# The last normalising turns of an attention stage moved behind the first matmuls of the next stage

## The chip, the core and the metric

The kernel runs on one core of a Trainium2 chip. The metric is the device time of one execution in microseconds (us). Engines of the core work side by side, each through its own queue in program order: TensorE (PE; its weight loads are shown apart as PEld), VectorE (DVE), ScalarE (ACT), GpSimd (POOL) and SyncE, which issues most DMAs (SPq). They wait for each other by semaphores.

## The reference

Three stages follow each other. Cut to what matters:

```
def _attn_ref(q, k, v, w1, b1, w2):          # 4 batches, 8 heads, 576 positions, 64 wide
    scores = scale * q @ k.T
    x = log1p(|i - j|) / log1p(max(i, 1))
    scores += (relu(x @ w1 + b1) @ w2)        # a bias for each head
    attn = exp(scores - max); attn /= sum(attn) + 1e-9
    return attn @ v
def _moe_ref(x, w_in, w_out):                 # 2304 tokens, 512 -> 2048 -> 512
    h = x @ w_in
    return (h - tanh(h)) @ w_out
def _moe2_ref(x, w_gate, w1, w2):             # one of 8 experts for each token
    e = argmax(x @ w_gate); g = softmax(x @ w_gate)[e]
    return g * (relu(x @ w1[e]) @ w2[e])
```

## The kernel before, in words

The three stages run in order: bias and attention, the dense layer with the routing, and the experts. The change lies in the attention stage and at its seam with the dense layer.

Attention works on 16 pairs of heads (`PAIRS_A`, pair `g`), each in 5 tiles of queries (`QT`; `rows(t)` is 128 for the first four and 64 for the last). For each step PE forms the scores of the next tile, turns the probabilities of this one by transposes into the PSUM banks `pt_a`, `pt_b` and `misc`, and multiplies those of an earlier pair with v into `o_acc` (`values_main`, `values_rest`). The output is kept transposed, so that queries lie along the free axis. The inverse row sums therefore have to be turned too: VectorE computes them (`inverse`, L665 and L667), repeats each over 64 columns (`widen`, L676, tile `at_inv_wide`), and PE transposes that tile by tile (`turn_inverse`, L464). VectorE multiplies the output copied from PSUM (`copy_main` L693, `copy_rest` L699, tile `at_o_sb`) with the turned inverses (`scaled`, L687) into `at_x_sb`, which SyncE stores to `x_dram`. The last pair has the number `LASTP`, 15. In the loop the turns of pair g come some steps later, one in each step; those of the last tile come once for each pair. After the loop the turns and products of the last two pairs stand written out.

The dense layer works on chunks of 384 tokens (`CH` is 3 tiles) and, within a chunk, on 16 slots m of 128 hidden columns. `up(m)` (L1009) is 12 matmuls of 384 columns into one of three banks, `down(m)` (L1054) is 9 matmuls of 512 columns. All operands are split in a high and a low half: `split_x_high` (ScalarE, L958) and `split_x_low` (VectorE, L963) for the tokens, `split_second_low` (L995) for a piece of the weights. Between `up` and `down` of a slot ScalarE squares (L1169, L1171), and takes the tanh and a mask (L1175, L1179); VectorE runs four operations (L1261, L1268, L1272, L1274), ScalarE takes the high half (L1185) and VectorE the low half (L1257). The seam is overlapped by hand: the attention function itself calls `dense.first_up`, which is `up(0)` and `up(1)`, at the end of its PE program, and the splits of the first chunk at the end of those of ScalarE and VectorE. The dense layer then issues `up(m+2)` ahead of `down(m)`. VectorE's first dense operation stands in its queue behind the two last `scaled` of pair 15.

SyncE at the seam, in its order: the store of pair 14, a piece of weights (`load_third_weights`), the second chunk of x, the store of pair 15 after the wait for its products (L385), a wait for all stores (L387), nine small loads and stores, and the next piece of weights (L935).

Of the kernel before, what the change touches and what calls it, by code (L numbers as in the profile page):

```python
# [26 lines left out]
P = 128  # L27
# [18 lines left out]
def rows(t):  # L46

    return P if t < QT - 1 else LAST
# [105 lines left out]
def bias_and_attention(nc, stay, mem, w1, b1, w2, dist, psi, rpsi_rows, bias_dram, q, k, v, ident, x_dram):  # L154
# [10 lines left out]
    with ExitStack() as ctx:  # L165
        def sem(name):
            return stay.enter_context(nc.semaphore("at_" + name))

        def buf(name, shape, dt=F32):
            return ctx.enter_context(nc.sbuf_tensor("at_" + name, shape, dt))  # L170
# [34 lines left out]
        id_sb, id_in = mem.id_sb, mem.id_in  # L205
# [4 lines left out]
        inv_wide = [buf(f"inv_wide{i}", [P, QT, 2 * D]) for i in range(2)]  # L210
# [24 lines left out]
        turn_done = sem("turn_done")  # L235
# [51 lines left out]
        def turn_of(g, t):  # L287

            p, tile = (g - 1, 0) if t == QT - 1 else (g - 2, t + 1)
            return (p, tile) if real(p) and g < PAIRS_A else None  # L290
# [98 lines left out]
        def tensor(pe, dense):  # L389
# [40 lines left out]
            def values(g, slot, o, at, queries):  # L430

                j_a, j_b = (slot, MID + 1 + slot) if slot < MID else (MID, MID)
                for c, j in ((0, j_a), (1, j_b)):
                    keys = slice(0, P) if j != MID else slice(c * D, (c + 1) * D)
                    last = nc.tensor.matmul(o[c * D:(c + 1) * D, at:at + queries.stop - queries.start],  # L435
                                            v_nat[g % NV][keys, j, :], prob_t[g % 2][keys, j, queries],
                                            start=slot == 0, stop=slot == MID)
                return last

            def values_main(g, slot):  # L440
                if slot == 0:
                    pe.wait_ge(v_in[g % NV], 16 * (g // NV + 1))
                    pe.wait_ge(pta_read, QT * g + QT - 1)
                    pe.wait_ge(ptb_read, QT * g + QT - 1)
                    pe.wait_ge(mid_read, QT * g + QT - 1)
                    if g:
                        pe.wait_ge(o_read, g)
                last = values(g, slot, o_acc, 0, slice(0, MAIN))
                if slot == MID:
                    last.then_inc(o_done, 1)  # L450

            def values_rest(g, bank, at):
                pe.wait_ge(pta_read, QT * (g + 1))
                pe.wait_ge(ptb_read, QT * (g + 1))
                pe.wait_ge(mid_read, QT * (g + 1))
                for slot in range(MID + 1):
                    last = values(g, slot, bank, at, slice(MAIN, S))
                last.then_inc(rem_done, 1)

            def turn_inverse(p, tile, bank, at):  # L460

                if tile == 0:
                    pe.wait_ge(widened, p + 1)
                nc.tensor.transpose(bank[:, at:at + P], inv_wide[p % 2][:, tile, :], id_sb[:, :]).then_inc(turn_done, 1)  # L464

            def misc_free(g, t):

# [19 lines left out]
            for g, t in STEPS:  # L487
                n = g * QT + t
                if real(g) and real((n + 1) // QT):
                    scores((n + 1) // QT, (n + 1) % QT)  # L490
                if not real(g):
                    continue
                pe.wait_ge(prob_done[0], n + 1)
                if n:
                    pe.wait_ge(pta_read, n)
                for j in range(MID):
                    last = turn_prob(pt_a, j * P, n, j)
                last.then_inc(pta_done, 1)
                if t == QT - 1:
                    values_main(g, 0)  # L500
                elif real(g - 1):
                    values_main(g - 1, t + 1)
                pe.wait_ge(prob_done[1], n + 1)
                if n:
                    pe.wait_ge(ptb_read, n)
                for j in range(MID + 1, KTP):
                    last = turn_prob(pt_b, (j - MID - 1) * P, n, j)
                last.then_inc(ptb_done, 1)
                misc_free(g, t)
                if turn_of(g, t):  # L510
                    turn_inverse(*turn_of(g, t), misc, TURN_AT)
                if t == QT - 1 and real(g - 1):
                    values_rest(g - 1, misc, REM)
                turn_prob(misc, 0, n, MID).then_inc(mid_done, 1)
# [3 lines left out]
            for tile in range(1, QT - 1):  # L518
                turn_inverse(LASTP - 1, tile, misc, tile * P)
            pe.wait_ge(pta_read, QT * PAIRS_A)  # L520
            turn_inverse(LASTP - 1, QT - 1, pt_a, 0)
            for slot in range(1, MID + 1):
                values_main(LASTP, slot)
            values_rest(LASTP, pt_b, 0)
            pe.wait_ge(x_done, QT * LASTP)
            for tile in range(QT - 1):
                turn_inverse(LASTP, tile, misc, tile * P)
            turn_inverse(LASTP, QT - 1, pt_a, 0)
            dense.first_up(pe)

        def scalar(act, dense):
            act.dma_start(dist_sb[:, :], dist).then_inc(dist_in, 16)
# [92 lines left out]
        def vector(dve, dense):  # L625
# [36 lines left out]
            def inverse(p):  # L662
                dve.wait_ge(prob_done[0], QT * (p + 1))
                dve.wait_ge(prob_done[1], QT * (p + 1))
                nc.vector.tensor_scalar_add(guarded[:, :, :], total[p % 2][:, :, :], 1e-9).then_inc(norm_step, 1)  # L665
                dve.wait_ge(norm_step, 2 * p + 1)
                nc.vector.reciprocal(inv[p % 2][:, :, :], guarded[:, :, :]).then_inc(norm_step, 1)  # L667

            def widen(p):

                dve.wait_ge(norm_step, 2 * p + 2)
                if p >= 2:
                    dve.wait_ge(turn_done, QT * (p - 1))
                one = inv[p % 2][:, :, :]
                many = bass.AP(one.tensor, one.offset, [one.ap[0], [1, 2 * QT], [0, D]])
                nc.vector.tensor_copy(inv_wide[p % 2][:, :, :].rearrange("p t (c d) -> p (t c) d", d=D), many).then_inc(widened, 1)  # L676

            def scaled(p, tile, tiles, bank, at):
                m = (tiles - 1) * P + rows(tile + tiles - 1)
                cols = slice(tile * P, tile * P + m)  # L680
                if tile <= 1 and p >= 2:
                    dve.wait_ge(x_out[p % 2], 16 * (p // 2))
                dve.wait_ge(turn_done, QT * p + tile + tiles)
                dve.wait_ge(o_read, p + 1)
                if tile + tiles == QT:
                    dve.wait_ge(rem_read, p + 1)
                nc.vector.tensor_tensor(x_sb[p % 2][:, cols], o_sb[:, cols], bank[:, at:at + m], ALU.mult).then_inc(x_done, tiles)  # L687

            def copy_main(p):
                if p:  # L690
                    dve.wait_ge(x_done, QT * p - 1)
                dve.wait_ge(o_done, p + 1)
                nc.vector.tensor_copy(o_sb[:, 0:MAIN], o_acc[:, :]).then_inc(o_read, 1)  # L693

            def copy_rest(p, bank, at):
                if p:
                    dve.wait_ge(x_done, QT * p)
                dve.wait_ge(rem_done, p + 1)
                nc.vector.tensor_copy(o_sb[:, MAIN:S], bank[:, at:at + LAST]).then_inc(rem_read, 1)  # L699
# [22 lines left out]
            for g, t in STEPS:  # L722
                n = g * QT + t
                m = rows(t)
# [22 lines left out]
                if turn_of(g, t):  # L747
                    p, tile = turn_of(g, t)
                    scaled(p, tile, 1, misc, TURN_AT)
                if t == QT - 1 and real(g - 1):  # L750
                    copy_rest(g - 1, misc, REM)
            for j in range(CH):
                dense.split_x_low(dve, 0, j)
            scaled(LASTP - 1, 1, QT - 2, misc, P)
            scaled(LASTP - 1, QT - 1, 1, pt_a, 0)
            inverse(LASTP)
            widen(LASTP)
            dense.split_second_low(dve)
            copy_main(LASTP)
            copy_rest(LASTP, pt_b, 0)  # L760
            scaled(LASTP, 0, QT - 1, misc, 0)
            scaled(LASTP, QT - 1, 1, pt_a, 0)

        return Attention(sync, tensor, scalar, vector, over, banks_read, turned)


# [4 lines left out]
CH = 3  # L771
# [1336 lines left out]
```

## Time and profile before

| what | us |
|---|---|
| device time, three runs | 1053.72, 1054.59, 1055.21 |
| median | 1054.59 |
| the profiled execution: device time | 1053.72 |
| its span, first to last instruction | 1051.8 |
| PE busy in the span | 1012.9 (96%) |
| VectorE, ScalarE busy | 689.2 (66%), 631.2 (60%) |

The 1.9 us between the span and the device time lie outside the first and last instruction. The attention stage reaches to about 346 us, the dense layer begins there. A busy PE means that a matmul is in its pipeline; in a stream of matmuls the distance of starts tells the pace, and the duration of one is longer than that distance.

### The profile page before, as it was taken

The numbers are of one execution on the slowest core, as the hardware profiler recorded it, in microseconds if no ns is written. First come the engines' busy times: TensorE is split into PE (matmuls) and PEld (weight loads), VectorE is DVE, ScalarE is ACT, GpSimd is POOL, SyncE is SP. The second block draws the span as 40 slices with busy tenths as digits, with TensorE's granted clock in tenths as the row PEclk, the third lists the DMA queues.
The fourth block names the chain that finished last, engine by engine and source line by source line (L and its number), as shares of the span: only waits on it lengthen the run. The fifth ranks groups of instructions, "written<-read, shape, count | busy, mean of one in ns | idle before, by whom it ended". The sixth has DMA issues, their size and how long they took to land. (4 is left out here: it accounts for less than half of the span.)

```text
span 1051.8 us, 19004 instructions
## 1 busy us (share of the span) xinstructions
PE 1012.9 (96%) x6540; PEld 787.9 (75%) x6540; DVE 689.2 (66%) x1570; ACT 631.2 (60%) x1340; POOL 87.3 (8%) x134
## 2 busy tenths in 40 slices
PE   6889999999999999999999999999998999999995
PEld 2256666666665789988988989888877888888884
DVE  7987878787888896766757657668754442632321
ACT  6987777777777685666566556567732432732421
POOL 0000000000000000000100100001023231331221
PEclk9999999999999999999999999999999999999998
DMA  7771252422512530010100100201115351631111
GB/s 227 265 250 56 71 168 71 160 81 65 148 46 94 183 111 1 31 31 31 31 1 31 31 1 31 81 31 58 40 51 205 122 195 40 215 102 40 36 40 36
DMA packets 62094, 92.15 MB, mean 88 GB/s; under 512 B 24486, under 2 KB 29990, under 8 KB 61990
## 3 DMA queue, kind: packets, MB, share of 16 engines
q1 hardware_dynamic: 56806, 79.32, 22.9%
q0 software_dynamic: 4192, 11.07, 3.3%
q8 instruction: 52, 0.85, 0.3%
q10 hardware_dynamic: 1008, 0.61, 0.2%
q14 instruction: 36, 0.29, 0.1%
HBM read 66.19 MB, written 25.73 MB: 87 GB/s over the span
## 5 line engine op out<-in xcount | busy, mean ns | idle before, releaser
L1009 PE MATMUL score<-dl_xt,dl_weights 128*128 128x384 f32 x1152 | 219.8, 339 | 0.0
L1009 PEld LDWEIGHTS score<-dl_xt,dl_weights 128*128 128x128 f32 x1152 | 202.1, 188 | 8.5 <-issue 3.0
L574 ACT ACTIVATE at_prob<-at_neg,at_negmax 128x576 f32<-128x576 f32 (+1 forms) x160 | 123.6, 773 | 54.2 <-DVE at_negmax L657 40.2
L1169 ACT ACTIVATE dl_val<-score 128x384 f32<-128x384 f32 x96 | 47.1, 490 | 131.3 <-PE score L1009 125.9
L1261 DVE SCALAR_TENSOR_TENSOR dl_sq<-dl_sq,dl_val 128x384 f32<-128x384 f32 x96 | 53.5, 557 | 99.3 <-ACT dl_sq L1171 97.7
L657 DVE CUSTOM_DVE_ANT_0 at_neg<-score,at_bias 128x576 f32<-128x576 f32 (+1 forms) x160 | 114.2, 750 | 2.2 <-PE score L420 1.7
L1814 PE MATMUL o_acc<-dl_weights,ex_ht_hi 128*128 128x512 f32 x336 | 109.1, 405 | 0.9 <-ACT ex_y_sb L1899 0.9
L1784 PE MATMUL score<-dl_weights,ex_xt_hi 128*128 128x512 f32 x336 | 105.6, 395 | 0.0
L435 PE MATMUL o_acc<-at_prob_t,at_v_nat 128*64 128x512 f32 (+1 forms) x320 | 85.7, 616 | 1.2 <-DVE at_o_sb L693 1.2
L428 PEld LDWEIGHTS pt_b<-id_sb,at_prob 128*128 128x128 f32 (+1 forms) x320 | 32.0, 140 | 63.5 <-ACT at_prob L574 48.1
L1479 POOL DMA_INDIRECT slot_dram<-slot_rows,slot_i x18 | 17.8, 987 | 727.5 <-DVE slot_i L1342 723.9
L1784 PEld LDWEIGHTS score<-dl_weights,ex_xt_hi 128*128 128x128 f32 x336 | 61.5, 188 | 12.2 <-issue 0.2
L1814 PEld LDWEIGHTS o_acc<-dl_weights,ex_ht_hi 128*128 128x128 f32 x336 | 60.0, 188 | 12.5 <-ACT ex_y_sb L1899 1.1
L1814 PE MATMUL o_acc<-dl_weights,ex_ht_lo 128*128 128x512 f32 x168 | 66.2, 394 | 0.0
L1784 PE MATMUL score<-dl_weights,ex_xt_lo 128*128 128x512 f32 x168 | 65.7, 391 | 0.0
L1054 PE MATMUL o_acc<-dl_weights,dl_g_hi 128*128 128x512 f32 x192 | 60.6, 396 | 1.9 <-DVE dl_g_lo L1257 1.6
L1171 ACT ACTIVATE dl_sq<-dl_val,minus_b 128x384 f32<-128x384 f32 x96 | 59.3, 618 | 3.1
L420 PE MATMUL score<-at_k_hi,at_q_hi 64*128 64x288 f32 x320 | 58.0, 340 | 2.6 <-DVE at_negmax L657 2.0
L1272 DVE COPY_PREDICATED dl_sq<-dl_over,dl_big 128x384 f32<-128x384 uint32 x96 | 57.8, 602 | 3.5 <-DVE dl_sq L1268 0.2
L1054 PE MATMUL score<-dl_weights,dl_g_hi 128*128 128x512 f32 x192 | 59.8, 392 | 0.0
L1054 PE MATMUL pt_b<-dl_weights,dl_g_hi 128*128 128x512 f32 x192 | 59.3, 390 | 0.0
L1179 ACT ACTIVATE dl_over<-dl_val,minus_small 128x384 f32<-128x384 f32 x96 | 58.2, 606 | 0.0
(222 smaller groups left out, 1985.8 us busy)
## 6 DMA issues: line engine op xcount, KB each, us to landing
dl_raw<-in_moe_w SPq DMA_DIRECT2D x12, 1024.0 KB, 7.6
ex_raw_b<-in_moe_w SPq DMA_DIRECT2D x8, 1024.0 KB
at_bias<-bias_dram SPq DMA_DIRECT2D x3, 2304.0 KB, 10.2
bias_dram<-at_prob SPq DMA_DIRECT2D x20, 288.0 KB, 2.1
at_k_all<-in_k SPq DMA_DIRECT2D x16, 288.0 KB, 3.5
at_q_all<-in_q SPq DMA_DIRECT2D x16, 288.0 KB, 4.2
at_v_nat<-in_v SPq DMA_DIRECT2D x16, 288.0 KB, 3.1
bias_dram<-at_rows_sb SPq DMA_DIRECT2D x16, 288.0 KB, 3.6
```

The lines of the kernel that those rows point to most:

```text
L420: last = nc.tensor.matmul(score[c][:, half, 0:HALF], a[g % 2][part, cols], b[g % 2][part, keys], start=i == 0, stop=i == 2)
L435: last = nc.tensor.matmul(o[c * D:(c + 1) * D, at:at + queries.stop - queries.start], v_nat[g % NV][keys, j, :], prob_t[g % 2][keys, j, qu ...
L574: nc.scalar.activation(prob[n % 2][0:m, c, :], neg[c][n % 2][0:m, :], ACT.Exp, bias=negmax[c][n % 2][0:m, 0:1], scale=-1.0, accum_out=tota ...
L657: nc.vector.tensor_tensor_reduce(out=neg[c][n % 2][0:m, :].rearrange("p (a c) -> p a c", a=2), in0=score[c][0:m, :, 0:HALF], in1=bias[hp % ...
L1009: last = nc.tensor.matmul(h_ps[m % NHB][:, 0:CN], w[f // KT][:, k, fc], x[c % 2][:, k, :], start=k == 0 and n == 0, stop=k == KT - 1 and n ...
L1054: last = nc.tensor.matmul(x2_ps[j][:, :], g[m % 2][:, tok], w[f // KT][:, f % KT, :], start=f == 0 and n == 0, stop=f == FT - 1 and n == 2)
L1171: nc.scalar.activation(sq[m % 2][:, :], val[m % 2][:, :], ACT.Square, bias=minus_b[:, 0:1], scale=SQ_A).then_inc(sq_done, 1)
L1179: nc.scalar.activation(over[m % 2][:, :], val[m % 2][:, :], ACT.Relu, bias=minus_small[:, 0:1]).then_inc(over_done, 1)
L1261: nc.vector.scalar_tensor_tensor(out=sq[m % 2][:, :], in0=sq[m % 2][:, :], scalar=SQ_C, in1=val[m % 2][:, :], op0=ALU.add, op1=ALU.mult).t ...
L1272: nc.vector.copy_predicated(s[:, :], over[m % 2][:, :].bitcast(mybir.dt.uint32), big[m % 2][:, :]).then_inc(dve_step, 1)
L1784: last = nc.tensor.matmul(h_ps[half][:, :], x[:, k, :], w1_of(r, half, w)[:, k, :], start=k == 0 and n == 0, stop=k == KT - 1 and n == 2)
L1814: last = nc.tensor.matmul(y_ps[:, :], x[:, half * KT + k, :], weights[:, r % 2, half, w, k, :], start=half == 0 and k == 0 and n == 0, sto ...
```

## The change

Three edits, all in `bias_and_attention`. `turn_inverse` transposes only the rows of the tile, so 64 by 64 of the identity for the last tile of a pair. `dense.first_up` stands before the turns of the last pair on PE. On VectorE the three `split_x_low` of the first chunk stand behind `widen(LASTP)`.

```
-                nc.tensor.transpose(bank[:, at:at + P], inv_wide[p % 2][:, tile, :], id_sb[:, :]).then_inc(turn_done, 1)
+                m = rows(tile)
+                nc.tensor.transpose(bank[:, at:at + m], inv_wide[p % 2][0:m, tile, :], id_sb[0:m, 0:m]).then_inc(turn_done, 1)
...
             values_rest(LASTP, pt_b, 0)
+            dense.first_up(pe)
             pe.wait_ge(x_done, QT * LASTP)
             for tile in range(QT - 1):
                 turn_inverse(LASTP, tile, misc, tile * P)
             turn_inverse(LASTP, QT - 1, pt_a, 0)
-            dense.first_up(pe)
...
-            for j in range(CH):
-                dense.split_x_low(dve, 0, j)
             scaled(LASTP - 1, 1, QT - 2, misc, P)
             scaled(LASTP - 1, QT - 1, 1, pt_a, 0)
             inverse(LASTP)
             widen(LASTP)
+            for j in range(CH):
+                dense.split_x_low(dve, 0, j)
             dense.split_second_low(dve)
```

PE's queue at the seam, before: the turns of pair 14, its last products with v, the turns of pair 15, then three `up`.

```order
L464 MATMUL misc<-id_sb,at_inv_wide 128x128 x3
L464 MATMUL pt_a<-id_sb,at_inv_wide 128x128
L435 MATMUL o_acc<-at_prob_t,at_v_nat 64x512 x8
L435 MATMUL pt_b<-at_prob_t,at_v_nat 64x64 x10
L464 MATMUL misc<-id_sb,at_inv_wide 128x128 x4
L464 MATMUL pt_a<-id_sb,at_inv_wide 128x128
L1009 MATMUL score<-dl_xt,dl_weights 128x384 x36
L1054 MATMUL o_acc<-dl_weights,dl_g_hi 128x512 x2
```

The same place now (line numbers behind the edit are one higher):

```order
L465 MATMUL misc<-id_sb,at_inv_wide 128x128 x3
L465 MATMUL pt_a<-id_sb,at_inv_wide 128x64
L435 MATMUL o_acc<-at_prob_t,at_v_nat 64x512 x8
L435 MATMUL pt_b<-at_prob_t,at_v_nat 64x64 x10
L1010 MATMUL score<-dl_xt,dl_weights 128x384 x24
L465 MATMUL misc<-id_sb,at_inv_wide 128x128 x4
L465 MATMUL pt_a<-id_sb,at_inv_wide 128x64
L1010 MATMUL score<-dl_xt,dl_weights 128x384 x12
```

Two of the three `up` (24 matmuls) stand ahead of the five turns of pair 15; the third stays behind them.

VectorE's queue at the seam, before. `dl_xt` is the low half of the tokens, `dl_sq` the first dense operation of slot 0.

```order
L699 COPY at_o_sb<-misc 128x64
L963 TENSOR_TENSOR dl_xt<-dl_x_nat,dl_xt 128x4x128 x3
L687 TENSOR_TENSOR at_x_sb<-at_o_sb,misc 128x384
L687 TENSOR_TENSOR at_x_sb<-at_o_sb,pt_a 128x64
L665 TENSOR_SCALAR at_guarded<-at_total 128x10
L667 RECIPROCAL at_inv<-at_guarded 128x10
L676 COPY at_inv_wide<-at_inv 128x640
L995 TENSOR_TENSOR dl_weights<-dl_raw,dl_weights 128x2048
L693 COPY at_o_sb<-o_acc 128x512
L699 COPY at_o_sb<-pt_b 128x64
L687 TENSOR_TENSOR at_x_sb<-at_o_sb,misc 128x512
L687 TENSOR_TENSOR at_x_sb<-at_o_sb,pt_a 128x64
```

The same place now, as far as the first dense operation of slot 0:

```order
L700 COPY at_o_sb<-misc 128x64
L688 TENSOR_TENSOR at_x_sb<-at_o_sb,misc 128x384
L688 TENSOR_TENSOR at_x_sb<-at_o_sb,pt_a 128x64
L666 TENSOR_SCALAR at_guarded<-at_total 128x10
L668 RECIPROCAL at_inv<-at_guarded 128x10
L677 COPY at_inv_wide<-at_inv 128x640
L964 TENSOR_TENSOR dl_xt<-dl_x_nat,dl_xt 128x4x128 x3
L996 TENSOR_TENSOR dl_weights<-dl_raw,dl_weights 128x2048
L694 COPY at_o_sb<-o_acc 128x512
L700 COPY at_o_sb<-pt_b 128x64
L688 TENSOR_TENSOR at_x_sb<-at_o_sb,misc 128x512
L1262 SCALAR_TENSOR_TENSOR dl_sq<-dl_sq,dl_val 128x384
```

The three `split_x_low` stand behind five attention operations. The two products of pair 15 keep their place ahead of the first dense operation.

## Rows read from the trace of the kernel before

**Rows 1.** The page: busy time, share of the span, instructions.
```profile
PE 1012.9 (96%) x6540; PEld 787.9 (75%) x6540; DVE 689.2 (66%) x1570; ACT 631.2 (60%) x1340; POOL 87.3 (8%) x134
```

**Rows 2.** Waits of PE after 350 us: total us, times, longest.
```profile
PE score L1797 <- DVE ex_h_sb L1965: 1.8, 1, 1.8
PE o_acc L1054 <- DVE dl_g_lo L1257: 1.6, 2, 0.9
PE misc L1773 <- DMA ex_x_sb<-x_dram,dl_tile_rows: 1.6, 2, 1.3
PE o_acc L1814 <- ACT ex_y_sb L1899: 0.9, 1, 0.9
```

**Rows 3.** Timeline of PE at the seam: start, duration, instructions, idle before.
```profile
340.44 0.52 PE L464 MATMUL misc<-id_sb,at_inv_wide 128*128 128x128 f32 x3 [0.97 <-DVE at_o_sb L699]
...
345.60 0.66 PE L464 MATMUL misc<-id_sb,at_inv_wide 128*128 128x128 f32 x4
346.09 0.27 PE L464 MATMUL pt_a<-id_sb,at_inv_wide 128*128 128x128 f32 x1
346.12 6.49 PE L1009 MATMUL score<-dl_xt,dl_weights 128*128 128x384 f32 x36
353.50 0.70 PE L1054 MATMUL o_acc<-dl_weights,dl_g_hi 128*128 128x512 f32 x2 [0.89 <-DVE dl_g_lo L1257]
```

**Rows 4.** Timeline of DVE at the seam.
```profile
339.96 0.22 DVE L699 COPY at_o_sb<-misc 128x64 f32<-128x64 f32 x1
340.27 1.90 DVE L963 TENSOR_TENSOR dl_xt<-dl_x_nat,dl_xt 128x512 fp32r<-128x512 f32 x3
342.09 0.55 DVE L687 TENSOR_TENSOR at_x_sb<-at_o_sb,misc 128x384 f32<-128x384 f32 x1
...
343.55 2.28 DVE L995 TENSOR_TENSOR dl_weights<-dl_raw,dl_weights 128x2048 fp32r<-128x2048 f32 x1
...
346.56 0.69 DVE L687 TENSOR_TENSOR at_x_sb<-at_o_sb,misc 128x512 f32<-128x512 f32 x1
347.17 0.21 DVE L687 TENSOR_TENSOR at_x_sb<-at_o_sb,pt_a 128x64 f32<-128x64 f32 x1
349.72 0.56 DVE L1261 SCALAR_TENSOR_TENSOR dl_sq<-dl_sq,dl_val 128x384 f32<-128x384 f32 x1 [2.34 <-ACT dl_sq L1171]
```

**Rows 5.** Timeline of ACT, first dense slot and two weights pieces.
```profile
348.55 0.49 ACT L1169 ACTIVATE dl_val<-score 128x384 f32<-128x384 f32 x1 [5.45 <-PE score L1009]
349.07 0.62 ACT L1171 ACTIVATE dl_sq<-dl_val,minus_b 128x384 f32<-128x384 f32 x1
...
356.27 1.91 ACT L1198 ACTIVATE dl_weights<-dl_raw 128x2048 fp32r<-128x2048 f32 x1
...
365.18 1.91 ACT L1200 ACTIVATE dl_weights<-dl_raw 128x2048 fp32r<-128x2048 f32 x1
```

**Rows 6.** Timeline of PE in the loop: turns of 128 and of 64.
```profile
282.13 0.27 PE L464 MATMUL misc<-id_sb,at_inv_wide 128*128 128x128 f32 x1
282.24 0.27 PE L428 MATMUL misc<-id_sb,at_prob 128*128 128x128 f32 x1
...
283.42 0.40 PE L428 MATMUL pt_a<-id_sb,at_prob 64*128 64x64 f32 x4
283.75 1.08 PE L435 MATMUL o_acc<-at_prob_t,at_v_nat 128*64 128x512 f32 x4
```

**Rows 7.** Groups of PEld by shape, 92 to 340 us: count, busy, mean ns.
```profile
L464 PEld LDWEIGHTS misc<-id_sb,at_inv_wide 128*128 128x128 f32 x71 | 9.9, 140 | 1.0
L428 PEld LDWEIGHTS pt_a<-id_sb,at_prob 64*128 64x128 f32 x56 | 5.5, 137 | 0.2 <-issue 0.2
```

**Rows 8.** SyncE's queue at the seam.
```profile
347.41 0.33 SPq L385 DMA_DIRECT2D x_dram<-at_x_sb  x1
352.21 0.37 SPq L1023 DMA_DIRECT2D dl_gate_sb<-in_moe_w_gate  x1
356.34 0.59 SPq L935 DMA_DIRECT2D dl_raw<-in_moe_w_in  x1
```

**Rows 9.** DMA issues 343 to 357 us: KB each, us to landing.
```profile
dl_raw<-in_moe_w_in SPq DMA_DIRECT2D x1, 1024.0 KB, 5.5
```

**Rows 10.** Windows: length, busy of PE, PEld, DVE, ACT, POOL, granted clock, DMA.
```profile
0.00:10.00 10.00, 1.51 (x10) 0.90 (x14) 4.87 (x20) 3.81 (x7) 0.21 (x5) 1.00 0.78 223
200.00:300.00 100.00, 99.77 (x842) 62.15 (x840) 79.74 (x242) 73.96 (x211) 0.00 (x0) 1.00 0.38 117
1045.00:1052.00 7.00, 0.00 (x0) 0.00 (x0) 0.00 (x0) 0.00 (x0) 0.00 (x0) 0.59 0.04 13
```

**Rows 11.** Timeline of PE, first idle time of the program.
```profile
9.07 5.81 PE L401 MATMUL score<-at_feat,at_w_blk 128*32 128x288 f32 x64 [2.19 <-DMA at_w_blk<-in_w]
```

More of the change, by code:

```diff
@@ L463, in turn_inverse @@
                     pe.wait_ge(widened, p + 1)
-                nc.tensor.transpose(bank[:, at:at + P], inv_wide[p % 2][:, tile, :], id_sb[:, :]).then_inc(turn_done, 1)
+                m = rows(tile)
+                nc.tensor.transpose(bank[:, at:at + m], inv_wide[p % 2][0:m, tile, :], id_sb[0:m, 0:m]).then_inc(turn_done, 1)
             def misc_free(g, t):
@@ L524, in tensor @@
             values_rest(LASTP, pt_b, 0)
+            dense.first_up(pe)
             pe.wait_ge(x_done, QT * LASTP)
@@ L528, in tensor @@
             turn_inverse(LASTP, QT - 1, pt_a, 0)
-            dense.first_up(pe)
         def scalar(act, dense):
@@ L751, in vector @@
                     copy_rest(g - 1, misc, REM)
-            for j in range(CH):
-                dense.split_x_low(dve, 0, j)
             scaled(LASTP - 1, 1, QT - 2, misc, P)
@@ L757, in vector @@
             widen(LASTP)
+            for j in range(CH):
+                dense.split_x_low(dve, 0, j)
             dense.split_second_low(dve)
```

## The prediction

> **What bounds the kernel now.** I read the page first: PE is busy 96% of the span [rows 1], and in the attention loop 99.77 of 100 us [rows 10]. So the time is PE's stream, and a change counts by what it takes out of that stream or by the holes it opens or closes in it. The waits of PE behind 350 us come next: a few us in all, and the one the change touches is `down(0)`, which waits for the low half of slot 0 from VectorE, 0.89 us at 353.50 [rows 2, 3]. The rest of the dense layer has almost no hole. The reader should then lay the timelines of the seam side by side. On PE the five turns of pair 15 start at 345.60 and `up(0)` at 346.12, 0.52 us later; three `up` run 6.49 us, to 352.61; PE then waits until 353.50 [rows 3]. On ScalarE the square of slot 0 starts at 348.55, after `up(0)` [rows 5]. On VectorE the last products of pair 15 end at 347.38, it sits idle 2.34 us, and the chain of slot 0 starts at 349.72 [rows 4]. The start of that chain sets `down(0)`: 353.50 - 349.72 = 3.78 us lie between them. What moves 349.72 moves everything behind it, since PE has no spare time there to catch up.
>
> **Part 1: `first_up` ahead of the turns.** `up(0)` starts where the turns did, 345.60, a gain of 0.52 us for the tokens' side: ScalarE's square would start at 348.03 and its second square would end at 349.69 - 0.52 = 349.17 [rows 5]. If VectorE were free, its chain would start 0.5 us earlier than before. It is not. The queue of VectorE is in program order, and ahead of its first dense operation stand the two products of pair 15, which need the turns. These now come after 24 matmuls. The pace of `up` is (6.49 - about 0.35 for the last one) / 35 = 0.175 us, so 24 take 4.2 us and the turns start at 345.60 + 4.2 = 349.8. The four into `misc` last 0.66 us [rows 3], to 350.45. With 0.05 us for the signal VectorE starts the large product at 350.5; the next one starts 0.61 us later (347.17 - 346.56), and the operation behind that about 0.13 us later (0.21 us long, overlapping its successor, as the small ones do) [rows 4]. The chain of slot 0 then starts at 350.5 + 0.61 + 0.13 = 351.24 in place of 349.72: 1.5 us late. `down(0)` comes at 351.24 + 3.78 = 355.0. PE has the same five turns and three `up` to do, ready at 352.6, so the hole of 0.89 us grows to 2.4 us. This term is +1.5 us, bounded by -0.5 (VectorE not held at all) and +1.8 (a signal of 0.2 us and a full 0.21 for the small product). I take +1.5.
>
> **Part 2: `split_x_low` later.** VectorE is free of the 128x64 copy at 340.18, but the product of pair 14 needs turns that PE starts at 340.44 and ends at 340.96 [rows 3, 4]. So it waits some 0.8 us, starts at 341.0 in place of 342.09, and the five small operations, which took 343.55 - 342.09 = 1.46 us, end at 342.5. The three splits (1.9 us) end at 344.4 in place of 342.17. `up(0)` needs them at 345.60: 1.2 us of cover. The split of the weights, 2.28 us, ends at 346.7, and the two copies behind it, which took from 345.83 to 346.56, at 347.5 [rows 4], under the wait for the turns at 350.5. SyncE gets pair 14 a microsecond earlier and the second load of x at about the same time as before. All of it is hidden; cost 0. If the cover were gone, each 0.1 us beyond 1.2 would delay `up(0)`, yet even then the order of events behind it is set by the turns, and they would shift with it.
>
> **Part 3: smaller turns.** Each of 16 pairs has one last tile; 14 of its turns lie in the loop, two at the end. Two 128-wide turns in the loop start 0.11 us apart, and four 64 by 64 turns of the same form take 0.33 us to the next group, 0.083 each [rows 6]. The difference is 0.03 us, and since PE is the bound there, it is time: 16 x 0.03 = 0.48, of which the one of pair 15 now lies ahead of the hole and gives nothing. I take -0.4. The ends are 0 (the load of weights binds) and 16 x 0.055 = -0.9 (the turn costs half).
> The loads of 64 rows last 137 ns where those of 128 last 140 [rows 7]. The Trainium skill, page "TensorE: Matmul & The Clock Gate", section "LDWEIGHTS (loading the stationary operand)", says that a load goes by its columns and not its rows, which these two rows bear out. It gives 107 ns for 128 columns; if that bound the turns, this term would be nothing and the sum +1.5. The 0.083 us of the 64 by 64 turns, which load 128 columns each, speaks against it as the binding limit.
>
> **Part 4: the store of pair 15.** It was issued at 347.41 and is now issued when its products end, at about 351.5. SyncE waited from there to 352.21 for it, 4.4 us and more, then took 4.13 us for nine small transfers and issued the next weights at 356.34 [rows 8], which landed 5.5 us later [rows 9], at 361.8. ScalarE needs them at 365.18 [rows 5], 366.7 when shifted. By the same waits again the weights would come at 351.5 + 4.8 + 4.1 + 5.5 = 365.9, still 0.8 us early, and probably earlier, since the large loads that the store queued behind are through by 351.5. Cost 0. ScalarE's own wait for all stores stands ahead of the weights at 356.27 [rows 5], about 357.8 now, and the store is in by 356.3 at worst.
>
> **Sum.** +1.5 - 0.4 = +1.1 us. Against the profiled execution, 1053.72, that is 1054.8. That execution was the fastest of three, 0.87 below the median, and the difference carries over to the median: 1054.59 + 1.1 = 1055.7.
>
> **Rivals.**
> - *The small turns save nothing*, by the weight load or because PE's instruction issue binds there. For it: the loads of weights last as long for 64 rows as for 128 [rows 7]. Against it: the 0.083 above. +1.5, so 1056.1.
> - *Given back later*: some later hole is set by something that doesn't move, a DMA or POOL, and takes up the 1.5 us. The holes of rows 2 name `ex_x_sb` from a gather, 1.6 us in all; but that gather waits for work that shifts with PE. Then only -0.4 is left: 1054.2.
> - *VectorE isn't held*, because the turns come through sooner than the queue suggests. The 0.5 us are gained and 0.4 on top: 1053.7. Against it: PE starts matmuls in the queue's order all along the timeline.
> - *Slower side, the clock falls in the wider hole.* The idle 2.19 us at the start passed at a granted clock of 1.00, level 2.4 GHz [rows 10, 11], and only the 7 idle us at the end show 0.59, so partly 1.2 GHz [rows 10]. The hole here would be 2.4 us with PE busy before it. It decides only if the wider hole makes the clock fall, which no row here tells. If one slot (`up` and `down`, 4.25 us from 353.50 to 357.75 in the loop's pace) ran at half the clock, it would add 4.2 us: 1059.9. The Trainium skill, same page, section "HAM oscillation — how this bites in real kernels", warns that idle gaps between bursts bring the slower level back.
> - *SyncE's queue is late*: the weights of part 4 miss the 0.8 us of cover by up to 1 us: 1056.7.
>
> **Chances.** The forecast 0.60, with 1054.8 to 1056.7 as its own range; small turns for nothing 0.15; given back 0.08; not held 0.05; clock 0.07; SyncE late 0.05. About 0.2% (2.1 us) is what a measurement of this kernel can tell from no change, so slower means above 1056.7 and faster below 1052.5. Slower: all of the clock's 0.07, 0.03 of SyncE's, 0.08 from the upper tails of the first two, 0.18. Faster: 0.04, tails of the third and fourth. The same: 0.78. The range, 1054.0 to 1057.3, leaves the clock and the outer tails out.
>
> **What would show it.** In the profile after: `up(0)` directly behind the last products with v at about 345.2 (0.4 less for the small turns); the turns of pair 15 between the second and third `up`; VectorE idle for about 3 us ahead of the product 128x512 with PE's turn named as what it waited for, and the chain of slot 0 right behind the small product with no wait for ScalarE; a hole of about 2.4 us before `down(0)`; the rest of the dense layer as before, shifted by 1.1 us. A hole under 1 us would refute the first term, `up(0)` starting still at 345.6 the third; PE's clock under 1.00 around 355 us would make the clock rival true.

## The result and the profile after

The changed kernel takes 1059.91 us (median of 5, 1058.96 to 1062.35) where the kernel before took 1054.59 (1053.72 to 1055.21). The ratio is 1.0053, 95% interval 1.0043 to 1.0064: slower by 5.3 us. The forecast was 1055.7, with a range of 1054.0 to 1057.3. The profiled execution took 1059.48 us, its span is 1057.6, 5.8 us over the span of before.

The timeline of PE at the seam shows where [rows 3]; columns as there. The third row is the last turn in the loop; before, it stood at 339.19.

```profile
338.46 0.27 PE L465 MATMUL misc<-id_sb,at_inv_wide 64*128 64x64 f32 x1
338.66 0.33 PE L428 MATMUL misc<-id_sb,at_prob 128*128 128x128 f32 x1
...
342.30 0.27 PE L428 MATMUL misc<-id_sb,at_prob 64*128 64x64 f32 x1
343.54 0.52 PE L465 MATMUL misc<-id_sb,at_inv_wide 128*128 128x128 f32 x3 [0.97 <-DVE at_o_sb L700]
...
348.80 4.44 PE L1010 MATMUL score<-dl_xt,dl_weights 128*128 128x384 f32 x24
353.07 0.60 PE L465 MATMUL misc<-id_sb,at_inv_wide 128*128 128x128 f32 x4
353.60 0.27 PE L465 MATMUL pt_a<-id_sb,at_inv_wide 64*128 64x64 f32 x1
353.81 2.35 PE L1010 MATMUL score<-dl_xt,dl_weights 128*128 128x384 f32 x12
358.37 0.70 PE L1055 MATMUL o_acc<-dl_weights,dl_g_hi 128*128 128x512 f32 x2 [2.21 <-DVE dl_g_lo L1258]
...
361.25 3.10 PE L1010 MATMUL score<-dl_xt,dl_weights 128*128 128x384 f32 x12
364.19 0.63 PE L1055 MATMUL o_acc<-dl_weights,dl_g_hi 128*128 128x512 f32 x2
```

The first turn of inverses in the loop, in the changed kernel and in the kernel before, and further rows of before:

```profile
93.67 0.33 PE L465 MATMUL misc<-id_sb,at_inv_wide 128*128 128x128 f32 x1
```
```profile
92.58 0.33 PE L464 MATMUL misc<-id_sb,at_inv_wide 128*128 128x128 f32 x1
...
339.19 0.27 PE L428 MATMUL misc<-id_sb,at_prob 64*128 64x64 f32 x1
...
355.64 2.27 PE L1009 MATMUL score<-dl_xt,dl_weights 128*128 128x384 f32 x12
357.75 0.63 PE L1054 MATMUL o_acc<-dl_weights,dl_g_hi 128*128 128x512 f32 x2
```

Read against the rows of before, four distances changed. The first turn of inverses in the loop starts at 93.67 and not 92.58: 1.1 us from the start of the program, which differs between executions. The kernel before and the one with the late splits alone, whose code is the same up to this turn, have it at 92.58 and 93.44. From that turn to the loop's last turn it is 248.63 us (93.67 to 342.30) where it was 246.61 (92.58 to 339.19): +2.0. From there to the first `down` it is 16.07 where it was 14.31: +1.8, with the hole grown from 0.89 to 2.21. And from the first `down` to the second it is 5.82 (358.37 to 364.19) where it was 4.25 (353.50 to 357.75): +1.6. The rows inside tell why: 12 matmuls of `up` last 3.10 us in place of 2.27. The windows give the granted clock there (the third value from the end, ahead of the DMA's two):

```profile
359.00:360.00 1.00, 1.00 (x6) 0.77 (x5) 0.97 (x3) 0.60 (x2) 0.00 (x0) 0.84 0.12 13
360.00:361.00 1.00, 1.00 (x4) 0.81 (x3) 0.88 (x3) 1.00 (x3) 0.00 (x0) 0.50 0.03 2
361.00:362.00 1.00, 1.00 (x5) 0.90 (x4) 0.97 (x2) 1.00 (x2) 0.00 (x0) 0.50 0.52 152
362.00:363.00 1.00, 1.00 (x5) 1.00 (x4) 0.60 (x2) 1.00 (x2) 0.00 (x0) 0.50 0.51 80
363.00:364.00 1.00, 1.00 (x7) 1.00 (x6) 0.83 (x1) 0.56 (x2) 0.00 (x0) 0.95 0.98 377
```

The clock fell to its lower level, 1.2 GHz, some 1.3 us after the hole's end (358.37; the window from 359 holds 0.84), and stayed there for some 3.4 us (0.16 + 3 x 0.50 + 0.05 = 1.7 us of lost clock). Behind the second `down` the rest of the program is 0.6 us shorter than before, no more than single executions differ.

VectorE's timeline answers to rows 4:

```profile
343.07 0.22 DVE L700 COPY at_o_sb<-misc 128x64 f32<-128x64 f32 x1
344.26 0.55 DVE L688 TENSOR_TENSOR at_x_sb<-at_o_sb,misc 128x384 f32<-128x384 f32 x1 [0.98 <-PE pt_a L465]
...
345.73 1.89 DVE L964 TENSOR_TENSOR dl_xt<-dl_x_nat,dl_xt 128x512 fp32r<-128x512 f32 x3
347.53 2.29 DVE L996 TENSOR_TENSOR dl_weights<-dl_raw,dl_weights 128x2048 fp32r<-128x2048 f32 x1
...
353.88 0.69 DVE L688 TENSOR_TENSOR at_x_sb<-at_o_sb,misc 128x512 f32<-128x512 f32 x1 [3.33 <-PE pt_a L465]
354.48 0.21 DVE L688 TENSOR_TENSOR at_x_sb<-at_o_sb,pt_a 128x64 f32<-128x64 f32 x1
354.62 0.55 DVE L1262 SCALAR_TENSOR_TENSOR dl_sq<-dl_sq,dl_val 128x384 f32<-128x384 f32 x1
```

It is held 3.33 us by PE's turn, and the chain of slot 0 starts right behind the two products, with no wait for ScalarE. The splits end at 347.62, 1.2 us ahead of `up(0)`.

### The profile page after: what moved, and what is told of

Same layout as the page of the kernel before. It is cut to its first block and busy times, and to the rows that moved or that the text cites. A ratio compares the mean times of both kernels' runs of the same rounds, so it can differ in the third digit from the quotient of the medians.

```text
span 1057.6 us, 19004 instructions
## 1 busy us (share of the span) xinstructions
PE 1018.5 (96%) x6540; PEld 790.7 (75%) x6540; DVE 689.2 (65%) x1570; ACT 631.5 (60%) x1340; POOL 88.8 (8%) x134
```

## The experiments

Times against the kernel before are differences of medians, with before run on the same chip beside them (1054.86, 1054.67 and 1054.86 us in the three series). "Loop" is the distance from the first turn of inverses to the last turn of the middle block, 246.61 us before; "seam" is from there to the first `down`, 14.31 us before.

**The small turns alone.** Only the first edit.

```
-                nc.tensor.transpose(bank[:, at:at + P], inv_wide[p % 2][:, tile, :], id_sb[:, :]).then_inc(turn_done, 1)
+                m = rows(tile)
+                nc.tensor.transpose(bank[:, at:at + m], inv_wide[p % 2][0:m, tile, :], id_sb[0:m, 0:m]).then_inc(turn_done, 1)
```

> The kernel before with only the 64 by 64 turns. Theory (the change of tile shape costs about 0.09 us on each side of a small turn): PE loses 0.14 to 0.15 us for each of 14 pairs in the loop, so +2.0 us against before, and the hole before the first down stays at 0.9 us with the clock at 1.00. Rival (the drift up to the seam in the changed kernel is the start of the execution, the small turns save what was forecast): 0 to -0.5 us.

Measured: 1057.06 us, +2.2, ratio 1.0018 (1.0009 to 1.0027). Loop 248.59 us (92.93 to 341.52), +2.0; the hole 0.89 us, the clock 1.00. The rival is out: less work on PE made the loop longer, by 0.14 us for each of the 14 small turns in it. The seam is 0.4 us longer as well, where two more small turns stand.

**The small turn at another place.** In the loop it stands behind the turn of the middle block, so that the scores, which use 64 rows, follow it. The semaphores that the two turns signal are exchanged with them.

```
...
-                if turn_of(g, t):
+                late = turn_of(g, t) and t == QT - 2
+                if turn_of(g, t) and not late:
                     turn_inverse(*turn_of(g, t), misc, TURN_AT)
...
-                turn_prob(misc, 0, n, MID).then_inc(mid_done, 1)
+                turn_prob(misc, 0, n, MID).then_inc(turn_done if late else mid_done, 1)
+                if late:
+                    turn_inverse(*turn_of(g, t), misc, TURN_AT, mid_done)
```

> The kernel before with 64 by 64 turns, where in the loop the small turn stands behind the turn of the middle block in place of ahead of it, so that its other neighbour is the scores, which work on 64 rows too. The two signals are exchanged with it. Theory (a change between 128 and 64 rows costs 0.09 us, and here the one to the scores is there anyway): within 0.7 us of before, the distance from the turn of the middle block to the scores longer by 0.05 us or less. Rival (a small turn is slow by itself, wherever it stands): +2.2 us as with the small turns alone.

Measured: 1055.28 us, +0.6, ratio 1.0005 (0.9996 to 1.0014). Loop 246.58 us (92.96 to 339.54): the 2.0 us are gone, with the same 64 by 64 turns. The seam is 16.39 us in the trace, 2.1 longer: 1.7 of it is a fall of the clock, shown in the last section, and 0.4 are the two small turns behind the loop, which stayed between wide ones.

Small turns aren't slow; their neighbours make them so. The starts of PE and of its weight loads (PEld) around one small turn show it. The changed kernel, with 128-row turns on both sides:

```profile
284.40 0.66 PE L428 MATMUL pt_b<-id_sb,at_prob 128*128 128x128 f32 x4
284.99 0.27 PE L465 MATMUL misc<-id_sb,at_inv_wide 64*128 64x64 f32 x1
285.19 0.33 PE L428 MATMUL misc<-id_sb,at_prob 128*128 128x128 f32 x1
285.45 0.40 PE L420 MATMUL score<-at_k_hi,at_q_hi 64*128 64x288 f32 x2
```
```profile
284.99 0.13 PEld L465 LDWEIGHTS misc<-id_sb,at_inv_wide 64*128 64x128 f32 x1 [0.17 <-issue]
285.19 0.14 PEld L428 LDWEIGHTS misc<-id_sb,at_prob 128*128 128x128 f32 x1
285.45 0.19 PEld L420 LDWEIGHTS score<-at_k_hi,at_q_hi 64*128 64x128 f32 x2
```

The kernel before at its counterpart of this place, PE and then PEld, where all the turns have 128 rows (the two turns behind this group are in [rows 6]):

```profile
281.64 0.66 PE L428 MATMUL pt_b<-id_sb,at_prob 128*128 128x128 f32 x4
...
282.55 0.40 PE L420 MATMUL score<-at_k_hi,at_q_hi 64*128 64x288 f32 x2
```
```profile
282.02 0.14 PEld L464 LDWEIGHTS misc<-id_sb,at_inv_wide 128*128 128x128 f32 x1
282.13 0.14 PEld L428 LDWEIGHTS misc<-id_sb,at_prob 128*128 128x128 f32 x1
```

Before, the load of a turn started at 282.02 and its matmul at 282.13: 0.11 us ahead, under the matmul in front. Between turns of different row counts the load starts together with its own matmul (284.99 and 284.99, 285.19 and 285.19), and the starts are 0.20 us apart in place of 0.11. The kernel before has such a step too, where scores of 64 rows follow a turn of 128: the turn starts at 289.54, the load and the first matmul of the scores both at 289.74. From the start of the group into `pt_b` to the scores it is 1.05 us where it was 0.91 (281.64 to 282.55); with the small turn behind the middle block it is 0.91 again (281.98 to 282.89). The Trainium skill ("TensorE: Matmul & The Clock Gate", "Part 3: Packing small matmuls — row/col tiling", The mechanism) states that a load overlaps with matmuls in flight "only when row_grp differs" (the group of rows that an instruction works on). In these traces the "only" doesn't hold: loads for equal 128-row tiles overlapped, and those between a 64-row and a 128-row tile, which share rows, didn't. The measurement decides.

**The two moves alone**, turns of 128 (second and third hunk of the change).

> The kernel before with only the two moves (first_up ahead of the turns of pair 15, the low splits behind widen), turns of 128. Theory (VectorE is held 1.5 us, and the clock falls in the wider hole): hole about 2.2 us, first down 1.3 to 1.8 us later, then about 3.4 us at a granted clock of 0.50, which costs 1.6 us more: +3.0 to +3.4. Rival (the clock's fall is not the hole's doing, or is no cost): +1.5. Rival (all of the loss is the order's): +5.3.

Measured: 1057.17 us, +2.3, ratio 1.0023 (1.0014 to 1.0032). Loop 246.64 us, seam 16.00, hole 2.47 us. The profiled execution kept its clock at 1.00. But the 11 executions form two groups: five from 1055.94 to 1056.33 us with a mean clock of 0.996 or 0.997, and six from 1057.17 to 1060.42 with 0.995 or 0.994. None of the three expectations is met as written. The lower group is +1.2 (median 1056.09), which is put down to the hole, and the upper one 1.5 more (median 1057.55), put down to a fall of the clock. That the upper six had a fall is inferred: only one execution of each kernel has a trace. The mean clock is a rough sign of it. The seven traces of this case without a fall before the end of the program show 0.996 or 0.997, the four with one show 0.996, so 0.996 can be either, and 0.995 is lower than any trace. Of the kernel before, run beside this one, 3 of 27 executions have 0.995 or less, of this kernel 6 of 11, of the changed kernel 16 of 30 (all its executions on record; the time above is the median of five).

**The late splits alone.** Only the third hunk.

> The kernel before with only the three low splits behind widen. Theory (they stay under the last products with v): 0, within 0.3 us, the first down as before and the hole 0.9 us. Rival (they delay the first up or the copies behind them and with them the chain of slot 0): +0.4 to +1.0 us, which would be part of what is put down to the moved turns.

Measured: 1054.70 us, -0.2, ratio 1.0000 (0.9991 to 1.0009); seam 14.31, hole 0.89. The splits are covered, and the 1.2 us belong to the moved turns.

**The turns between the first two `up`**, 128 wide, splits late. `first_up` takes the number of the `up` here.

```
+            dense.first_up(pe, 0)
             pe.wait_ge(x_done, QT * LASTP)
             for tile in range(QT - 1):
                 turn_inverse(LASTP, tile, misc, tile * P)
             turn_inverse(LASTP, QT - 1, pt_a, 0)
-            dense.first_up(pe)
+            dense.first_up(pe, 1)
```

> The kernel before with the low splits behind widen and the five turns of pair 15 (128 wide) between up(0) and up(1). Theory (the loss of the order is VectorE held by the products of pair 15 until the turns are through): up(0) starts 0.5 us earlier than before, the products run from about 0.8 us after the end of up(0), the chain of slot 0 starts 0.4 to 0.5 us earlier relative to the last products with v, the hole before the first down is 0.3 to 0.5 us, the clock stays at 1.00: -0.3 to -0.5 us, a difference that can hardly be told. Rival (the late splits or the moved up cost something of their own): +0.5 to +1.5.

Measured: 1053.96 us, -0.7, ratio 0.9996 (0.9987 to 1.0005): not to be told from before. In the trace the seam is 13.91 us, 0.4 shorter. VectorE now waits 1.15 us and not 3.33:

```profile
348.65 0.69 DVE L688 TENSOR_TENSOR at_x_sb<-at_o_sb,misc 128x512 f32<-128x512 f32 x1 [1.15 <-PE pt_a L464]
349.26 0.21 DVE L688 TENSOR_TENSOR at_x_sb<-at_o_sb,pt_a 128x64 f32<-128x64 f32 x1
349.39 0.55 DVE L1261 SCALAR_TENSOR_TENSOR dl_sq<-dl_sq,dl_val 128x384 f32<-128x384 f32 x1
```
```profile
353.16 0.70 PE L1054 MATMUL o_acc<-dl_weights,dl_g_hi 128*128 128x512 f32 x2 [0.41 <-DVE dl_g_lo L1257]
```

One `up` more or less ahead of the turns is the difference between a gain of 0.4 us at the seam and a loss of 1.7.

The clock did fall in this profiled execution, though not at the seam but in the expert stage, behind an idle time of 1.76 us. The rows of this kernel, its window, and the rows of before, where the same idle time passed at 1.00:

```profile
796.50 0.66 PE L1797 MATMUL score<-id_sb,ex_h_sb 128*128 128x128 f32 x4 [1.76 <-DVE ex_h_sb L1965]
...
804.66 0.66 PE L1773 MATMUL misc<-id_sb,ex_x_sb 128*128 128x128 f32 x4 [0.22 <-DMA ex_x_sb<-x_dram,dl_tile_rows]
```
```profile
798.00:801.00 3.00, 3.00 (x9) 2.33 (x8) 0.52 (x1) 0.00 (x0) 1.04 (x1) 0.50 1.00 369
```
```profile
796.93 0.66 PE L1797 MATMUL score<-id_sb,ex_h_sb 128*128 128x128 f32 x4 [1.76 <-DVE ex_h_sb L1965]
...
804.53 0.66 PE L1773 MATMUL misc<-id_sb,ex_x_sb 128*128 128x128 f32 x4 [1.27 <-DMA ex_x_sb<-x_dram,dl_tile_rows]
```

From the first of these rows to the last it is 8.16 us where it was 7.60, so this fall cost 0.6 us: PE's next wait, for a gather, shrank from 1.27 to 0.22 and gave the rest back.

**A hole in the kernel before.** Its own order, and VectorE kept busy by 5 more copies ahead of `copy_main(LASTP)`.

```
+            dve.wait_ge(o_done, PAIRS_A)
+            dve.wait_ge(x_done, QT * LASTP)
+            for n in range(5):
+                nc.vector.tensor_copy(o_sb[:, 0:MAIN], o_acc[:, :]).then_inc(held, 1)
+                dve.wait_ge(held, n + 1)
             copy_main(LASTP)
```

> The kernel before in its own order, with 5 copies of 128x512 added on VectorE ahead of copy_main(LASTP), some 3.3 to 3.6 us, of which 2.3 are covered. Theory: the hole before the first down grows to about 2.0 to 2.3 us with no other change, and the clock falls as in the changed kernel: +1.1 to +1.4 for the hole and +1.6 for the clock, together +2.8. Rival (it takes the moved turns to bring the clock down): clock 1.00 and +1.2.

Measured: 1056.98 us, +2.1, ratio 1.0016 (1.0007 to 1.0025). Seam 15.50, hole 2.05 us, clock 1.00 in the profiled execution, and again two groups: five executions from 1055.45 to 1056.15 with 0.996 or 0.997, and six from 1056.98 to 1058.74, four of these with 0.995, the others with 0.996 and 0.998. The first group is +0.6, its median 1055.46. So a hole of this size gives the same picture without the moved turns, less clearly: four of the six later executions have a mean clock lower than any trace, and the one with 0.998 must be late for another reason.

**The hole filled**, in the changed kernel and in the one with the two moves alone.

```
                     attention.banks_read(pe)
+                    for n in range(9):
+                        nc.tensor.matmul(x2_ps[0][:, :], win_hi[0][:, n % KT, 0:P], win_hi[0][:, n % KT, :], start=True, stop=True)
```

> The changed kernel with 9 matmuls of 512 columns put in the hole before the first down (about 2.0 us of PE work whose result is overwritten), nothing else. Theory (PE's idle time makes the clock fall): the granted clock stays at 1.00 behind 355 us and the time is 1.5 us under the changed kernel, so +3.7 against before. Rival (the clock falls for another reason, as the small turns or the phase of the execution): clock 0.50 for 3.4 us again and +5.3. Rival (the filling itself delays down): above +5.3.

Measured: 1058.63 us, +3.8, ratio 1.0035 (1.0022 to 1.0049); four of the five executions lie between 1058.45 and 1058.71, and none has a mean clock under 0.996. PE's row shows the filling and no idle time ahead of `down`, and the window behind it the clock at 1.00:

```profile
355.80 2.25 PE L1099 MATMUL o_acc<-dl_weights 128*128 128x512 f32 x9
357.98 0.73 PE L1055 MATMUL o_acc<-dl_weights,dl_g_hi 128*128 128x512 f32 x2
```
```profile
356.00:364.00 8.00, 8.00 (x38) 6.66 (x37) 7.06 (x13) 6.73 (x12) 0.00 (x0) 1.00 0.36 99
```

Nine matmuls whose result is thrown away make the changed kernel 1.3 us faster (1059.91 to 1058.63). None of its own 30 executions is under 1058.86.

> The two moves with turns of 128, as in the order-only kernel, and 10 matmuls of 512 columns in the hole before the first down (about 2.2 us of work whose result is overwritten). Theory (the fall of the clock comes from PE's idle time there, and comes only in part of the executions): the upper group of the order-only kernel (1057.2 and above, mean clock 0.994 to 0.995) is gone, all executions lie near its lower group, +1.2 to +1.5 us. Rival (the two groups come from something else): the same two groups again, 1.3 us apart.

Measured, with ten: 1056.42 us, +1.6, ratio 1.0015 (1.0006 to 1.0024). Nine of the 11 executions lie between 1055.63 and 1056.71; one of the 11 has a mean clock under 0.996, where it was six. Two are slower, 1057.48 and 1058.90, with 0.996. The first of these is the profiled one: its clock is 1.00 from 340 to 1040 us, and PE waits 3.1 us for the gather `ex_x_sb` where it was 1.6 [rows 2]. So the low-clock executions became rare with the hole filled, and single executions can be late for another reason.

**Both mended**, small turns behind the middle block and the last turns between the `up`.

> The two of this series together: small turns behind the turn of the middle block in the loop, and the turns of pair 15 between up(0) and up(1). Theory: the sum of the two, -1.0 to +0.2 us against before, no fall of the clock before the end. Rival (small turns slow by themselves): +1.7.

Measured: 1054.22 us, -0.5, ratio 0.9997 (0.9988 to 1.0006). Loop 246.62 us (92.69 to 339.31), seam 14.27, hole 0.41. Its profiled execution has a fall of the clock near 798 us as well, behind an idle time of 1.77 us. This and the turns between alone are the best of the series; neither beats the kernel before by more than the measurement can tell.

## Why the prediction was wrong

- **Part 1, `first_up` ahead of the turns: right.** Forecast +1.5 us with a hole of 2.4; measured 2.21 us of hole in the changed kernel, a seam longer by 1.7 us with the two moves alone, and +1.2 (their lower group) to +1.6 (hole filled) in the time. The mechanism is the one told: VectorE's queue holds the chain of slot 0 behind two products that wait for PE. Moving one `up` to the other side of the turns takes it away.
- **Part 2, late splits: right.** 0, and 1.2 us of cover as worked out.
- **Part 3, smaller turns: this step failed.** It stood at -0.4 with ends of 0 and -0.9, and is +2.0 in the loop and +2.2 alone. The error is in how the number was made. 0.083 us was read from four 64 by 64 turns in a row, and used for one that stands between 128-row turns. A place of before pointed the other way: four 64-row turns into `pt_b` are followed by a 128-row one, and to that turn it is 0.39 us, where the same four ahead of a product of `values_main` take 0.33 [rows 6]. And the 0.33 itself holds a step between unlike tiles: one of these four lasts 0.22 us and all of them 0.40, so their starts are 0.06 us apart, and the step from the last one to the product is 0.15. Divided by four, the dear step was hidden in a mean of 0.083.

```profile
284.76 0.46 PE L428 MATMUL pt_b<-id_sb,at_prob 64*128 64x64 f32 x4
285.15 0.33 PE L464 MATMUL misc<-id_sb,at_inv_wide 128*128 128x128 f32 x1
```

  A bound that allowed only a gain had no row to exclude the loss. The rule on loads that was weighed there bore on the length of a load, 137 against 140 ns [rows 7], and not on when it may start.
- **Part 4, the store of pair 15: right.** Issued at 354.72, the next weights at 360.98 and no wait for them.
- **The clock rival: the right mechanism, given 0.07 and mis-sized.** It happened in the profiled execution of the changed kernel and, by the mean clock, in many of those with a hole of 2.05 or 2.47 us. One slot at half clock was priced at 4.2 us; measured it is 1.3 to 1.6. That this rival's 1059.9 is the measured time is luck: 2.7 us too much for the clock stand against 2.6 us too little for the small turns (2.2 in place of -0.4). The idle 2.19 us at a granted clock of 1.00 [rows 11] was taken as evidence that such a hole is harmless. The two-move kernel shows that one execution can't say that: its profiled one came through 2.47 us at 1.00, and six others of the same program were later, with a lower mean clock.
- **The sum.** Small turns 2.2, held chain 1.2, clock about 1.5: 4.9 of the measured 5.3 us (interval 4.5 to 6.8).

## What to carry to other kernels

A transpose that uses fewer rows than its neighbours can cost more than a full one: put it beside work on the same rows, and read the distance of starts at the place itself, not in a row of equals. Where work is pulled ahead on one engine, look in the other engines' queues for what waits behind the work that now comes later. Keep PE from idling ahead of a long stretch of matmuls, and judge such a hole by many executions. A fall of the clock costs less where PE has to wait again soon.

## What the runs showed of the hardware

In four of the eleven traces the granted clock fell to 0.50 for about 3.4 us in the middle of the program. In the changed kernel this came after a hole of 2.21 us, at a cost of 1.6 us in the trace and 1.3 us between the times with and without the filling. Holes of 2.47 and 2.05 us passed at 1.00 in the traces of the two moves and of the added hole; that other executions of these two fell is inferred from their mean clock. In the two kernels with the turns between the `up` it fell after 1.76 and 1.77 us, and the same code with the same idle time passed at 1.00 in the trace of before; with PE's wait for a DMA close behind in before, the fall cost 0.6 and 0.2 us. It can fall after less: in the profiled execution of the small turns at another place, PE is idle 0.68 us at 337 and 0.97 us before 340.79, and the products behind take 5.50 us where they took 3.80:

```profile
340.79 0.52 PE L465 MATMUL misc<-id_sb,at_inv_wide 128*128 128x128 f32 x3 [0.97 <-DVE at_o_sb L703]
...
341.44 5.50 PE L435 MATMUL o_acc<-at_prob_t,at_v_nat 128*64 128x512 f32 x16
```
```profile
340.00:350.00 10.00, 9.21 (x53) 4.58 (x54) 7.64 (x15) 3.43 (x5) 0.00 (x0) 0.83 0.60 193
```

The kernel with both mended has the same code up to there and the same idle times, 0.68 and 0.97 us, and passed at 1.00, with 3.80 us for the products. The kernel before has nearly the same (0.64 and 0.97), so part of its own spread (1053.88 to 1056.77 us in 27 executions beside that series) may be this; that wasn't tried. The Trainium skill ("TensorE: Matmul & The Clock Gate", "HAM oscillation — how this bites in real kernels") warns of idle gaps between bursts, and the trace of the changed kernel agrees, with 0.50 behind a gap of 2.21 us; the 2.47 us at 1.00 show that such a gap doesn't always do it. Why an execution falls and the next does not stays open.
